# Attention of a fused attention and mixer kernel: fp32 products over 64 rows of TensorE in place of split fp32r products over 128 rows

## What is computed

```python
batch, n_heads, seq, head_dim = 4, 8, 576, 64
q_rot, k_rot = rotate(q), rotate(k)            # 32 + 32 halves of a row, by cos and sin
scores = (1 / sqrt(64)) * q_rot @ k_rot.T      # 576 x 576 for each of 32 heads
attn = exp(scores - max(scores))
attn = attn / (sum(attn) + 1e-09)
x = (attn @ v) as (batch, seq, 512)
h = relu(x.T @ w_tok1) @ w_tok2                # token mixing, width 256
u = x + h.T
out = u + relu(u @ w_ch1) @ w_ch2              # channel mixing, width 1536
```

## Time and profile before

| | us |
|---|---|
| median of 3 runs | 639.42 (639.29 to 639.71) |
| the profiled execution, its own time | 639.26 |
| its span in the profile | 637.4 |
| busy PE / PEld / DVE / ACT / POOL over the span | 621.5 / 604.5 / 509.9 / 465.2 / 341.4 |

### The profile page before, as it was taken

How to read it: one execution, slowest core, us unless ns; L and a number is a source line. 1 busy time by engine, 2 the same in 40 slices (tenths; PEclk the granted TensorE clock), 3 DMA queues, 4 the chain that set the end, 5 groups by cost and what they waited for, 6 DMA issues and landing times.

```text
span 637.4 us, 13799 instructions
## 1 busy us (share of the span) xinstructions
PE 621.5 (98%) x4724; PEld 604.5 (95%) x4724; DVE 509.9 (80%) x881; ACT 465.2 (73%) x1018; POOL 341.4 (54%) x316
## 2 busy tenths in 40 slices
PE   4899999999999999999999999999999999999997
PEld 3799999999999999999999999999999999999997
DVE  7899999999999999977385985569935499553895
ACT  5888999988888999976383655776556765567753
POOL 4999999998888887551900002860017800068200
PEclk9999999999999999999999999999999999999999
DMA  4667766676668765406002331000320003100002
GB/s 130 177 152 205 199 161 169 170 188 172 168 180 212 206 172 127 110 20 217 20 1 64 136 99 60 1 2 2 84 75 0 0 0 82 48 27 2 0 3 74
DMA packets 59594, 62.32 MB, mean 98 GB/s; under 512 B 16592, under 2 KB 43856, under 8 KB 59536
## 3 DMA queue, kind: packets, MB, share of 16 engines
q1 hardware_dynamic: 59232, 61.50, 35.4%
q10 hardware_dynamic: 304, 0.07, 0.0%
HBM read 30.77 MB, written 9.44 MB: 63 GB/s over the span
## 4 chain that ended last, share of the span: by engine, by line
PE 95%; DVE 1%; POOL 1%; ACT 1%; issue 0%
PE slot L624 12%; PE rest L657 12%; PE rest L634 9%; PE slot L1359 8%; PE slot L1361 8%; PE slot L1360 8%; PE rest L1359 6%; PE rest L1361 6%; PE rest L1360 6%; PE rest L383 3%; PE rest L585 3%; PE rest L644 2%; PE slot L1391 2%; PE rest L1391 2%; PE rest L224 1%; PE rest L221 1%
## 5 line engine op out<-in xcount | busy, mean ns | idle before, releaser
L1350 POOL TENSOR_TENSOR w_ch_part<-w_ch_sums,w_ch_part 128x512 fp32r<-128x512 f32 x21 | 31.0, 1476 | 173.3 <-ACT w_ch_part L1603 173.3
L997 DVE TENSOR_REDUCE neg_max<-slot 128x1 f32<-128x576 f32 x142 | 106.7, 752 | 6.3 <-PE slot L624 2.0
L1667 ACT ACTIVATE pieces<-h 128x288 fp32r<-128x288 f32 x168 | 73.8, 444 | 49.8 <-PE slot L1361 24.5
L1005 DVE TENSOR_TENSOR pt_lo<-rest,pt_hi 128x512 fp32r<-128x512 f32 x144 | 96.0, 677 | 1.8 <-ACT pt_hi L854 1.3
L657 PE MATMUL rest<-pt_hi,v 128*128 128x256 f32 (+1 forms) x320 | 89.3, 303 | 0.0
L854 ACT ACTIVATE pt_hi<-rest 128x512 fp32r<-128x512 f32 x144 | 84.1, 596 | 5.1 <-PE rest L634 4.2
L1758 DVE TENSOR_TENSOR pieces<-h,pieces 128x288 fp32r<-128x288 f32 x168 | 74.4, 453 | 9.3 <-ACT pieces L1667 8.8
L657 PE MATMUL rest<-pt_lo,v 128*128 128x256 f32 (+1 forms) x256 | 69.7, 295 | 0.0
L847 ACT ACTIVATE prob_a<-slot,neg_max 128x576 f32<-128x576 f32 x78 | 57.9, 743 | 9.8 <-DVE neg_max L997 9.6
L624 PE MATMUL slot<-key,q_hi 128*128 128x288 f32 x252 | 63.5, 333 | 1.5 <-ACT prob_a L847 0.5
L657 PEld LDWEIGHTS rest<-pt_hi,v 128*128 128x128 f32 x320 | 60.3, 188 | 0.2
(11 more groups left out here) (268 smaller groups left out, 2109.3 us busy)
## 6 DMA issues: line engine op xcount, KB each, us to landing
key<-t_hi_k SPq DMA_DIRECT2D x31, 144.0 KB, 2.3
key<-t_lo_k SPq DMA_DIRECT2D x31, 144.0 KB, 2.4
raw_qk<-in_q_dram SPq DMA_DIRECT2D x16, 256.0 KB, 2.6
raw_v<-in_v_dram SPq DMA_DIRECT2D x16, 256.0 KB, 3.1
x_scratch<-x_pair SPq DMA_DIRECT2D x16, 256.0 KB, 2.2
stage_or_x<-x_scratch SPq DMA_DIRECT2D x16, 256.0 KB, 4.1
q_hi<-t_hi_q SPq DMA_DIRECT2D x31, 128.0 KB, 2.4
q_cross<-t_hi_q SPq DMA_DIRECT2D x31, 128.0 KB, 2.4
```

The costliest lines, as they stand in the source:

```text
L997: dve.tensor_reduce(neg_max[p % 2][:, i:i + 1], slot[g if 2 <= g < 4 else g % 2][:, :, 0:HALF], AX.XY, ALU.max, negate=True).then_inc(maxe ...
L1005: dve.tensor_tensor(pt_lo[:, :, cols], rest[:, bank, :].rearrange("p (j n) -> p j n", j=G), f32(pt_hi[:, 0:G, cols]), ALU.subtract).then_i ...
L1667: act.activation(pieces[:, ring(m), 0, :], source[WEIGHTS[n]][:, ft, :], ACT.Copy).then_inc(piece_hi, 1)
```

## The change

All matmuls of the attention take 64 rows (partitions 0 to 63 or 64 to 127) and full fp32 operands; pairs of such matmuls, one on each half of the rows, stand next to each other in the order and write different PSUM banks.

- There are no high and low parts of q, k, v or the probabilities any more. ACT copies the turned q (with the scale), DVE the turned k. A copy moved to the other 64 partitions (`moved_x`) is made by 4 DMAs a pair in place of 10.
- Scores: for an ordinary tile 2 matmuls of 288 columns, keys 0 to 287 on one half of the rows and 288 to 575 on the other; 4 for the shared tile.
- Turn: each tile by 10 half transposes (5 key blocks x 2 halves of the queries) into the two banks `rest[:, 0:2]`. ACT copies what stands in the first (`copy_up`), DVE the second (`copy_low`), 320 columns each; the next turn waits for both. The tails are padded by zeros to a fifth block.
- Products with v: the turned probabilities are the weights (64 rows x 128 queries), v with a column of ones streams (65 columns): 9 matmuls for each ordinary tile, 18 for the shared one, 90 a pair, into `rest[:, 2:4]`. The result has queries on partitions, so nothing is turned back; its 65th column is the sum, so the exponential accumulates none. DVE adds the two banks (`sum_o`), adds the epsilon (`guard`, on POOL before) and inverts, once for each head.
- Turned k and q of the next pair use the score slots; rotated k and q have two buffers each. POOL copies v (`copy_v`, one instruction for each head in place of two).
- Everything of pair p but its last three tiles is done in step p; `last_o` and `last_sums` in the mixer go.

The diff, cut to its core:

```diff
     def tensor(pe):
+        def half_turn(to, x, r):
+            rows = (top, low)[r]
+            return pe.matmul(to, x, ident[rows, rows], start=True, stop=True, is_transpose=True, skip_group_check=True)
...
-            for t in range(NG):
-                to = first_q(t * P, (t + 1) * P) if n == "q" and p == 0 else columns(bank, W)[:, t * P:(t + 1) * P]
-                mm = pe.transpose(to, rot[n][:, t].rearrange("p h d -> p (h d)"), ident[:])
+            for t in range(NG):
+                x = rot[n][p % 2][:, t].rearrange("p h d -> p (h d)")
+                for r in range(2):
+                    mm = half_turn(to[:, r, t * D:(t + 1) * D], x[(top, low)[r]], r)
...
-                passes = ((q_hi[a][:, cols], key[a]), (q_cross[a][:, cols], key[a]))
-            for n, (queries, keys) in enumerate(passes):
-                for f in range(2):
-                    mm = pe.matmul(s[:, f, 0:HALF], queries, keys[:, f * HALF:(f + 1) * HALF],
-                                   start=(n == 0), stop=(n == len(passes) - 1))
+                for r, (x, w) in enumerate((own(0), other(1)) if a == 0 else (other(0), own(1))):
+                    mm = pe.matmul(s[:, r, 0:HALF], x[:, cols], w, start=True, stop=True, skip_group_check=True)
...
-            pe.wait_ge(exped, p * TILES + i + 1)
-            for j in range(G):
-                mm = pe.transpose(rest[:, bank, j * P:(j + 1) * P], prob[i][:, j * P:(j + 1) * P], ident[:])
+                pe.wait_ge(up_done, g)
+                pe.wait_ge(low_done, g)
+            pe.wait_ge(exped, g + 1)
+            for j in range(NG):
+                for r, rows in enumerate((top, low)):
+                    at = j * P if j < G or (i in UPPER and (i, r) != (G, 0)) else S - P
+                    x = wide[i][rows, at:at + P]
+                    mm = half_turn(rest[:, r, j * D:(j + 1) * D], x, r)
...
-            for j in range(NG):
-                for pt in ((pt_hi, pt_lo) if j < G else (pt_hi,)):
-                    mm = pe.matmul(rest[:, PV_BANK[f], 0:n1 - n0], v_sb[a][:, j, :], pt[:, j, n0:n1],
-                                   start=(j == 0 and pt is pt_hi), stop=(j == NG - 1))
+            def add(r, n, x, w, j, begins=False, ends=False):
+                rows = (top, low)[r]
+                at = (n - HEADS["AB"[n >= G]][0]) * V
+                return pe.matmul(rest[:, 2 + r, at:at + V], x[rows, j, :], w[rows, j, :], start=begins, stop=ends, skip_group_check=True)
...
+            elif i in (0, 2, 5, 7):
+                for j in range(G):
+                    add(0, i, pt_of(p, i), v_sb[a], j, begins=(j == 0), ends=(j == G - 1))
+                    add(1, i, pt_of(p, i), v_sb[a], j, begins=(j == 0))
+                return
+            else:
+                add(1, i - 1, pt_of(p, i - 1), v_sb[a], G, ends=True).then_inc(o_added, 1)
+                add(0, i, pt_of(p, i), v_sb[a], G, begins=True)
+                for j in range(G):
+                    add(0, i, pt_of(p, i), v_sb[a], j, ends=(j == G - 1))
+                    mm = add(1, i, pt_of(p, i), v_sb[a], j, begins=(j == 0), ends=(j == G - 1))
...
     def scalar(act, h1_of_batch_0):
-            act.activation(pt_hi[:, 0:G, i * P:(i + 1) * P], rest[:, bank, :].rearrange("p (j n) -> p j n", j=G),
-                           ACT.Copy).then_inc(hi_done, 1)
+            act.activation(to[:, :, top], rest[:, 0, 0:NG * D].rearrange("p (j n) -> p j n", j=NG), ACT.Copy).then_inc(up_done, 1)
...
     def vector(dve):
-            dve.tensor_tensor(pt_lo[:, :, cols], rest[:, bank, :].rearrange("p (j n) -> p j n", j=G),
-                              f32(pt_hi[:, 0:G, cols]), ALU.subtract).then_inc(lo_done, 1)
+            dve.tensor_copy(to[:, :, low], rest[:, 1, 0:NG * D].rearrange("p (j n) -> p j n", j=NG)).then_inc(low_done, 1)
```

More of the change, by code:

```diff
@@ L277, in attention @@
+    rot["q"][0] = sb(ctx, "rot_q0", [P, NG, 2, D])
     raw["v"] = sb(ctx, "raw_v", [P, 2, NG, D])
[L278 to L282, removed]
+    prob_b = sb(ctx, "prob_b", [P, G * S + 2 * TAIL])
+    starts = {0: 0, 1: S, 2: 2 * S + TAIL, 3: 3 * S + TAIL, G: 4 * S + 2 * TAIL, 5: 0, 6: S, 7: 2 * S + TAIL, 8: 3 * S + TAIL}
@@ L612, in score, with own, other @@
+            queries, keys = (turned_x[n][p % 2] for n in "qk")
+            def own(r):
+                rows = (top, low)[r]
+                return queries[rows], keys[rows, r * HALF:(r + 1) * HALF]
+            def other(r):
+                rows = (top, low)[r]
+                return moved_x["q"][rows], moved_x["k"][rows, :]
             if i == G:
-                cols, b = slice(MAIN, W), p % 2
-                passes = ((t_hi["q"][b][:, cols], t_hi["k"][b]), (t_hi["q"][b][:, cols], t_lo["k"][b]),
-                          (t_lo["q"][b][:, cols], t_hi["k"][b]))
+                cols = slice(MAIN, W)
+                for n, halves in enumerate(((own(0), other(1)), (other(0), own(1)))):
+                    for r, (x, w) in enumerate(halves):
+                        mm = pe.matmul(s[:, r, 0:HALF], x[:, cols], w, start=(n == 0), stop=(n == 1), skip_group_check=True)
@@ L635, in turn, with values @@
             mm.then_inc(turned, 1)
[L637 removed]
+        def values(p, i):
             if no(p):
                 return
[L641 to L659 removed]
@@ L728, in tensor @@
+            mm.then_inc(o_added, 1)
+        pe.wait_ge(consts, 2)
+        transposes("k", 0)
+        transposes("q", 0)
+        for p in range(N):
+            score(p, 0)
+            turn(p - 1, 7)
+            values(p - 1, 6)
             score(p, 1)
-            after_sum(p - 2, "B")
-            transpose_o(p - 2, "A")
+            turn(p - 1, 8)
+            values(p - 1, 7)
             score(p, 2)
-            after_lo(p - 1, 4)
-            values(p - 1, "A0", 2, 1)
-            after_sum(p - 2, "A")
@@ L1517, in body @@
                 u_unit(b, c, begins)
-                if begins and c == 0:
-                    first.last_o(pe)
             if begins:
```

732 lines of the change are left out of this document (260 added, 472 removed).

## The result

The changed kernel takes 677.16 us (median of 4 runs, 677.07 to 677.72) against 639.56 us before: the ratio is 1.059, 95% interval 1.057 to 1.061. It is slower by 37.6 us; the forecast was 668 us in a range of 600 to 715, with 0.61 for slower.

The account below looks back on a forecast made before the run. TensorE's stream and VectorE were both taken to bound the 17.16 us pair. Scores 5.2, half transposes 3.4, products 9.9 and waits 0.5 make 19.0 us; over 16 pairs +29 on 639.3 gives 668 us, range 600 to 715.

Parts of the forecast that it names:

- the first rival: Products with v: weight loads hide under streaming and VectorE sets the pair at 14.9 us; 603 us, chance 0.33.
- (a) Streaming: TensorE's plain fp32 matmuls: time per streamed column, bounds 0.84 to 1.8 ns, taken as 1.8.
- (b): Weight loads of a plain fp32 product with v: from one of 0.062 us to two of 0.11, taken as two of 0.11.
- (c) Side by side: Neighbouring TensorE matmuls on different halves of the rows: taken to overlap fully, so each term halves.
- Products with v: TensorE in the attention: 90 products set by two loads of 0.11 us, 9.9 us a pair against 4.77 before.
- half transposes: TensorE's turns of tiles, q and k: 110 under a load of 0.062 us, 3.4 us a pair against 6.9.
- scores: TensorE's score matmuls: 20 a pair, 5.2 us against 4.94 before, no gain.
- Waits: TensorE's waits in a pair: left at today's 0.5 us because the new order gives each chain room.
- Loads hidden, VectorE next: Products with v fall to 5.3 us a pair and VectorE sets the pair at 14.9; 603 us, chance 0.33.
- Side by side fails: TensorE's two halves take turns, so nothing halves: 27.7 to 37 us a pair, about 810 to 957 us; 0.20 including the load-waits rival's 0.05.
- a load waits for its own half's matmul: On each half of TensorE's rows load and stream add: 26.8 us a pair, 793 us; chance 0.05.
- In between: TensorE neighbours overlap but start in order, idling a half: +1.6 us a pair, 612 or 694 us; mixtures near no change 0.07.

Follow-up runs that it names:

- the fp32r runs: Changed kernel with turned probabilities and v kept as fp32r, low parts left out: 620.06 us; the same with tile 3's score ahead of the first product: 616.38 us.
- more columns: Changed kernel with 96 columns of v streamed past each block of turned probabilities in place of 65: 676.77 us.
- half the weights: Changed kernel with only 64 of each block's 128 queries loaded as weights of the products with v: 639.71 us.
- the early score: Changed kernel with the score of tile 3 ahead of a pair's first product with v on TensorE, not behind it: 668.32 us.
- the run with halves in turn: Changed kernel with each tile's products with v ordered four blocks on one half of the rows, then four on the other: 769.51 us.
- three runs that introduce one: Changed kernel with 64 queries as weights: 639.71 us; with products of 128-key blocks over all rows: 718.67; with ordinary tiles' turns over all rows: 735.75.

## Why the prediction was right

**What bounds the kernel.** That a change must lighten both TensorE's stream and VectorE wasn't tried one at a time. What was seen fits: lighter work for VectorE alone, with a longer stream, lost; and the fp32r runs, in which both are lighter, are the ones that came clearly below 17.16 us a pair (15.6). The page's clock was read as full everywhere; ahead of 14.4 us the durations say that it wasn't, as above. One size was off: I added up mean durations of VectorE's instructions, 14.3 us, and set the sum against a busy time in which neighbours' overlap is counted once. Its busy time after is 12.99 us, while nine maxima of 0.756, nine copies of 0.48 and the rest add to about 14 as forecast. This touched only the first rival.

**The three unknown prices.** (a) Streaming: a pass of 288 columns takes 0.24 to 0.25 us (203.32 - 203.07), two passes 1.7 ns a column; I had taken 1.8 and the upper bound. (b) Two loads of 0.112 us each, as taken: no gain from more columns, 5 us a pair from half the weights or from one load. (c) Side by side: yes, with starts 0.04 us apart. The fork that decides the sign was (b), and the row that decided it, the fp32r load of the earlier trace rows, was the right neighbour: a plain fp32 product loads like an fp32r one, twice, and not like a transpose.

**The terms.** Products with v 10.0 us a pair (forecast 9.9), half transposes 11 x 0.31 = 3.4 (3.4), scores about 5.3 (5.2): 18.7 for 18.5. Waits: 0.7 by the starts, 0.5 taken, and for another reason than the waits of before, so that the size came near was luck. I had checked the chain from score to exponential, which does have room, and overlooked the banks of the products: one head's sums must be read before the next head's products begin. The rows of the fp32r run name it, and the early score returns 0.46 us a pair. In all 19.36 for 19.0, 6 us over 16 pairs; and outside the regular pairs 2.7 us, within the 3 that I had allowed for the start and end, but in part for a late rise of the clock that I hadn't thought of. These make up nearly all of the 9 us between 668 and 677.

**The rivals.** *Loads hidden, VectorE next* (603 us) failed on its condition, and the fp32r run, whose products cost 5.0 us a pair where this rival had 5.3, shows about what it would have been: 616 to 620, since the copies of turned probabilities hold TensorE before VectorE is full. *Side by side fails* and *a load waits for its own half's matmul* are out by the steps: 0.112 us a pass is the load alone. (The Trainium skill, "TensorE: Matmul & The Clock Gate", The mechanism, says that a load overlaps a running matmul only where the row groups differ. These runs don't agree: here a pass of one half starts every 0.112 us, with an estimated 0.054 us of streaming in it (65 columns at the 0.84 ns of a pass of 288), and the two don't add; over all 128 rows it is 0.112 us too.) *In between* had it that neighbours start in order, so that a half idles for up to a pass at each change of length (8 times up to 0.23 us is up to 1.8 us a pair, not 1.6; its two times would lie up to 4 us higher). The trace shows passes of the two halves alternating, and the run with halves in turn shows one half ahead of the other by several matmuls, which a start in order would not allow.

**A cost that I hadn't priced** is a change of the array's shape, about 0.15 us in three runs that introduce one (0.12 to 0.13 if one leaves out that the wait before the first product shrank in the same runs). The change avoids it by keeping all matmuls of the attention at 64 rows x 128 columns. (The Trainium skill, "TensorEngine Tiling (Array Packing)", Key Properties, says that a change of tiling mode drains the engine, without a figure; these runs agree.) The 0.15 us also give an estimate of what half transposes alone would bring in a kernel whose other matmuls have 128 rows, which wasn't tried: 0.31 in place of 0.54 us a tile saves 0.23, and two changes cost 0.30, so nothing.

## What to carry to other kernels

Where the streamed side is narrow, count weight loads, not matmuls or columns: at 65 columns past 128 weights a plain fp32 product costs its two loads, and splitting it over halves of the rows gives nothing that one matmul over all rows wouldn't. The kernel before had v as the weights and streamed the wide operand, in three fp32r products of parts; that took 4.8 us a pair for 10.1. How much of this is the order of the operands and how much the number format wasn't tried: an estimate for plain fp32 with the wide operand streaming over halves of the rows is 9 blocks x 576 queries x 2 passes x 0.84 ns = 8.7 us a pair (two heads, two halves side by side), so most of the gap would remain. And before lightening the engines around TensorE, ask what it costs in TensorE's own steps: relief of 3.6 us a pair on VectorE was bought with 2.2 us on the engine that sets the end.

## What the runs showed of the hardware

- Halves of the rows act like two queues: each takes its own matmuls in order, and one runs ahead of the other by several matmuls when the program lists them in groups.
- A plain fp32 matmul runs as two passes with a load each, and the passes of two neighbours alternate (202.78, 202.81, 203.07, 203.11), so pairs on two halves overlap in full.
- A change of shape between 64 x 128 and 128 x 128, or 64 x 64, costs about 0.15 us (three runs).
- A weight load runs beside the streaming of the matmul before it even over the same rows: full-row passes of 65 columns start every 0.112 us, which is the load's step alone.
- With one half idle for much of the time the granted clock fell to 1.2 GHz for 48 us, and for six shorter times, each time within 1.1 us of the end of a wait of 0.5 us. The changed kernel, with the same waits but both halves at work, kept its clock. Whether the idle half is the cause, or it together with the wait, wasn't tried by itself; it was the only run whose products were grouped by half, and the only profiled one that lost the clock in the attention once it had risen.
- The rise to 2.4 GHz came 9 us later than before (23.6 for 14.4 us), behind waits of 0.73 and 0.24 us that the kernel before doesn't have there; in the other variants of the changed kernel it came at 19.7 to 24.7 us. What sets the moment isn't shown.
